# Attention, token mixing and gated net on one core: the token product of the gated net from seven products of quarters, and the work around it in another order

## The reference, cut to what matters

```python
def _moe2_ref(x, w_in, w_spatial, b_spatial, w_out):   # x: 4 x 768 x 384
    h = np.maximum(x @ w_in, 0.0)                       # w_in: 384 x 1024
    u, v = h[..., :512], h[..., 512:]
    v_n = (v - mean(v)) / sqrt(var(v) + 1e-06)          # over the last axis
    v_s = np.einsum('ts,bsd->btd', w_spatial, v_n) + b_spatial[None, :, None]
    return (u * v_s) @ w_out                            # w_out: 512 x 384
```

## Time and profile before

| | us |
|---|---|
| median of 3 runs (lowest, highest) | 599.46 (597.94, 602.70) |
| profiled execution, its own time | 600.73 |
| its span in the profile | 599.0 |
| granted TensorE clock, mean share of full | 0.992 |
| TensorE busy | 582.9 (97%) |
| VectorE busy | 360.4 (60%) |
| ScalarE busy | 283.8 (47%) |

### The profile page before, as it was taken

How to read it: one execution, slowest core, us unless ns; L and a number is a source line. 1 busy time by engine, 2 the same in 40 slices (tenths; PEclk the granted TensorE clock), 3 DMA queues, 4 the chain that set the end, 5 groups by cost and what they waited for, 6 DMA issues and landing times.

```text
span 599.0 us, 11967 instructions
## 1 busy us (share of the span) xinstructions
PE 582.9 (97%) x4248; PEld 557.9 (93%) x4248; DVE 360.4 (60%) x595; ACT 283.8 (47%) x493; POOL 61.4 (10%) x102
## 2 busy tenths in 40 slices
PE   6899999999999999999999999999999999999997
PEld 3788888899999999999999999989999999999996
DVE  6799999677685567447653786555065605570250
ACT  5699999755564244424533635125322523162111
POOL 6366556000000000000000000000000000000000
PEclk9799999999999999999999999999999999999999
DMA  8979999276002130221033540200120010001102
GB/s 192 214 230 244 258 250 337 86 265 250 8 33 63 61 116 13 66 72 48 13 119 127 212 163 2 79 2 1 69 90 1 0 53 26 1 1 40 40 0 82
DMA packets 31115, 58.77 MB, mean 98 GB/s; under 512 B 3680, under 2 KB 23136, under 8 KB 30688
## 3 DMA queue, kind: packets, MB, share of 16 engines
q1 hardware_dynamic: 30816, 57.62, 32.0%
q10 hardware_dynamic: 256, 0.59, 0.4%
HBM read 44.04 MB, written 14.16 MB: 97 GB/s over the span
## 4 chain that ended last, share of the span: by engine, by line
PE 74%; DVE 3%; issue 2%; ACT 1%; DMA 1%; DVEq 0%; ACTq 0%
PE gate_ps L1121 17%; PE theta_bank L1121 11%; PE ringc L1121 11%; PE small_ps L1121 10%; PE mix_ps L1587 8%; PE mix_ps L1592 8%; PE mix_ps L1588 8%; PE small_ps L1551 1%; DVE stats L2119 1%; DVE w_lo L82 1%; DMA x2T<-x 1%; PE mix_ps L1121 1%; DVE vn L2137 0%; DVE x L1785 0%; ACT w_hi L77 0%
## 5 line engine op out<-in xcount | busy, mean ns | idle before, releaser
L1587 PE MATMUL mix_ps<-w_hi,z_hi 128*128 128x384 f32 x288 | 98.6, 342 | 0.0
L1588 PE MATMUL mix_ps<-w_lo,z_hi 128*128 128x384 f32 x288 | 96.6, 336 | 0.0
L1592 PE MATMUL mix_ps<-w_hi,z_lo 128*128 128x384 f32 x288 | 73.5, 337 | 0.0
L1121 PE MATMUL gate_ps<-w_hi 128*128 128x384 f32 x192 | 64.2, 334 | 0.0
L1121 PE MATMUL gate_ps<-w_hi,w_lo 128*128 128x384 f32 x192 | 64.2, 334 | 0.0
L1121 PE MATMUL gate_ps<-w_lo,w_hi 128*128 128x384 f32 x192 | 64.1, 334 | 0.0
L77 ACT ACTIVATE g_hi<-gate 128x384 fp32r<-128x384 f32 x32 | 16.9, 527 | 81.6 <-DVE gate L2169 81.6
L2165 DVE TENSOR_TENSOR gate<-gate_ps,b_all 128x384 f32<-128x384 f32 x32 | 17.8, 557 | 62.5 <-PE gate_ps L1121 62.5
L1587 PEld LDWEIGHTS mix_ps<-w_hi,z_hi 128*128 128x128 f32 x288 | 54.1, 188 | 0.1
L1588 PEld LDWEIGHTS mix_ps<-w_lo,z_hi 128*128 128x128 f32 x288 | 54.2, 188 | 0.0
L1592 PEld LDWEIGHTS mix_ps<-w_hi,z_lo 128*128 128x128 f32 x288 | 51.9, 188 | 0.3 <-DVE z_lo L82 0.3
(11 more groups left out here) (166 smaller groups left out, 1398.9 us busy)
## 6 DMA issues: line engine op xcount, KB each, us to landing
v_raw<-in_vC_dram SPq DMA_DIRECT2D x16, 288.0 KB, 4.9
xT<-y_sb SPq DMA_DIRECT2D x32, 144.0 KB, 4.3
xt<-xT SPq DMA_DIRECT2D x8, 576.0 KB, 4.0
w_raw<-in_wB_dram SPq DMA_DIRECT2D x6, 768.0 KB, 5.7
u<-xT SPq DMA_DIRECT2D x8, 576.0 KB, 5.0
x2T<-x SPq DMA_DIRECT2D x24, 192.0 KB, 1.9
xt<-x2T SPq DMA_DIRECT2D x8, 576.0 KB, 4.7
out_dram<-y SPq DMA_DIRECT2D x24, 192.0 KB, 1.9
```

The costliest lines, as they stand in the source:

```text
L1121: done = pe.matmul(out, a, b, start=(first and n == 0), stop=(last and n == len(terms) - 1))
L1587: pe.matmul(out, z, w_hi[:, weights_of[r]], start=(s == 0 and r == 0), stop=False)
L1588: pe.matmul(out, z, w_lo[:, weights_of[r]], start=False, stop=False)
L1592: last = pe.matmul(out, part(z_lo[i], r * DMODEL + d * 128, 128), w_hi[:, weights_of[r]], start=False, stop=(s == ST - 1 and r == 1))
```

## The change

The product over tokens is cut in halves of tokens in, halves of tokens out and halves of the 512 features, and made of seven products of quarters (the Winograd form of one level of Strassen) where it was eight. `PRODUCTS` names them: each is a values operand (768 columns: 3 token tiles x 256 features) by a weights operand (1152 columns: 3 token tiles x 384). For each product and each 128 features (m) TensorE issues 3 x 3 matmuls of 384 columns into one bank: 7 x 2 x 9 = 126 matmuls for a batch.

- The operands that are sums are made on VectorE: four differences of weights once (`combine`, at the end of the token mixing), four sums of values for each batch (`combine_first_half`, `combine_halves`).
- The values are normalised into one tile, and split only after their sums are there: seven splits of 768 columns on each of ScalarE and VectorE, where there were six of 512. The tile of raw values is the place of their hi parts or lo parts.
- VectorE adds the products up out of PSUM with 22 additions per batch (`add`, bias included), where there were 8, and 8 multiplications by `ut` in place.
- TensorE's order is v(b), output(b-1), u(b), spatial(b), and u sits in the ring's banks after output. ScalarE puts the outputs between the splits of the values, and all of u behind them.
- The next x is loaded into the place of its lo part once u has been made, and split within `gates`; the splits of the gates come after all gates (in the last batch between them).
- The weights for it are loaded in quarters earlier, and four of their eight splits move into the gated net.

```diff
+QUARTER = ST // 2 * HALF
+OPERAND = ST // 2 * FH // 2
+OUT_COLS = FT * DMODEL
+W_AT = {name: n * QUARTER for n, name in enumerate(("t4", "b11", "t1", "b22", "b21", "t3", "t2", "out"))}
+W_ORDER = ("b11", "t2", "b21", "t3", "t1", "t4", "b22", "out")
+V_AT = {name: n * OPERAND for n, name in enumerate(("a11", "s1", "a12", "a22", "s3"))}
+V_TAIL = W_AT["out"] + OUT_COLS
+V_ORDER = ("a11", "s3", "s2", "a12", "s1", "a22", "s4")
+PRODUCTS = (("a11", "b11"), ("s2", "t2"), ("a12", "b21"), ("s3", "t3"), ("s1", "t1"), ("a22", "t4"), ("s4", "b22"))
+SUMS = 22
...
+    def load(self, sp, wC, name):
+        if name == "out":
+            sp.dma_start(self.w_raw[:, self.cols("out")], wC[:, WC_OUT:WC_OUT + OUT_COLS]).then_inc(self.raw_in[name], 16)
+            return
+        s_half, t_half = int(name[1]) - 1, int(name[2]) - 1
+        tokens = wC[:, WC_SP + s_half * ST // 2 * SEQ:WC_SP + (s_half + 1) * ST // 2 * SEQ].rearrange("p (s t) -> p s t", t=SEQ)
+        at = self.cols("t1" if name == "b12" else name)
+        sp.dma_start(self.w_raw[:, at].rearrange("p (s t) -> p s t", t=HALF), tokens[:, :, t_half * HALF:(t_half + 1) * HALF])\
+          .then_inc(self.raw_in[name], 16)
...
+    def difference(self, dve, out, a, b):
+        raw = lambda name: self.w_raw[:, self.cols(name)]
+        dve.tensor_tensor(raw(out), raw(a), raw(b), ALU.subtract).then_inc(self.combined, 1)
+    def combine(self, dve):
+        for name in ("b12", "b22", "b11", "b21"):
+            dve.wait_ge(self.raw_in[name], 16)
+        self.difference(dve, "t3", "b22", "t1")
+        dve.wait_ge(self.combined, 1)
+        self.difference(dve, "t1", "t1", "b11")
+        dve.wait_ge(self.combined, 2)
+        self.difference(dve, "t2", "b22", "t1")
+        dve.wait_ge(self.combined, 3)
+        self.difference(dve, "t4", "b21", "t2")
...
+            def load_spatial(name):
+                def f(b):
+                    if last_batch(b):
+                        if name == "out":
+                            sp.wait_ge(mix_done.h, mix_done.at(b, GROUPS))
+                        else:
+                            sp.wait_ge(mix_used.h, mix_used.at(b, {"b11": 1, "b12": 2, "b22": 3, "b21": 3}[name]))
+                        spatial.load(sp, wC, name)
+                return f
...
+                batches(sp, [(load(0), 0), (load_spatial("out"), 2), (store(0), 2), (load_spatial("b11"), 1), (store(1), 2), (store(2), 2),
+                             (load_spatial("b12"), 1), (load(1), 0), (load_x2, 1), (store(3), 2), (load_spatial("b22"), 1),
+                             (load_spatial("b21"), 1), (store(4), 2), (store(5), 2), (load_residual, 1), (load_w_in, 1)], 2, 1)
...
+            def w_c_combine(b):
+                if last_batch(b):
+                    dve.wait_ge(theta_ps.h, theta_ps.at(b, ST))
+                    dve.wait_ge(mix_used.h, mix_used.at(b, 5))
+                    spatial.combine(dve)
...
-                    (z_down(5), 1), (reduce(0), 0), (multiply(0), 0),
+                    (z_down(5), 1), (w_c_combine, 1), (reduce(0), 0), (multiply(0), 0),
...
+            def value_up(n):
+                name = V_ORDER[n]
+                def f(b):
+                    act.wait_ge(vn_done.h, vn_done.at(b, ST // 2 if name == "a11" else ST))
+                    if name in ("s3", "s1", "s2", "s4"):
+                        act.wait_ge(combined.h, combined.at(b, ("s3", "s1", "s2", "s4").index(name) + 1))
+                    act.wait_ge(vs_ps.h, vs_ps.at(b.back(1), vs_ps.per))
+                    split_hi(act, value_hi(name), value_raw(name)).then_inc(vhi_done.h, 1)
...
+                for o in range(GATES):
+                    act.wait_ge(gated.h, gated.at(b, o + 1))
+                    split_hi(act, g_hi[:, gate_cols(o)], ut[:, gate_cols(o)]).then_inc(ghi_done.h, 1)
+                    if o in (1, 3) and not last_batch(b):
+                        x_hi(b.back(-1), o // 2)
...
-                (v_out(2), 1), (deviation(1), 1), (vn_up(0), 1),
-                (v_out(3), 1), (deviation(2), 1), (vn_up(1), 1),
-                (v_out(4), 1), (deviation(3), 1), (vn_up(2), 1),
-                (v_out(5), 1), (deviation(4), 1), (vn_up(3), 1), (u_out(0), 1), (deviation(5), 1), (vn_up(4), 1),
-                (u_out(1), 1), (vn_up(5), 1), (u_out(2), 1), (u_out(3), 1),
-                (u_out(4), 1), (u_out(5), 1), (u_out(6), 1), (u_out(7), 1),
-                (y_out, 2), (x_hi, 0), (gate_up, 1)], 2)
+                (v_out(2), 1), (deviation(1), 1), (w_up(4), 1),
+                (v_out(3), 1), (deviation(2), 1), (w_up(5), 1),
+                (v_out(4), 1), (deviation(3), 1), (w_up(6), 1),
+                (v_out(5), 1), (deviation(4), 1), (deviation(5), 1),
+                (value_up(0), 1), (y_out(0), 2), (value_up(1), 1), (y_out(1), 2), (value_up(2), 1), (y_out(2), 2),
+                (value_up(3), 1), (y_out(3), 2), (value_up(4), 1), (y_out(4), 2), (value_up(5), 1), (y_out(5), 2), (value_up(6), 1),
+                (u_out(0), 1), (u_out(1), 1), (u_out(2), 1), (u_out(3), 1),
+                (u_out(4), 1), (u_out(5), 1), (u_out(6), 1), (u_out(7), 1), (w_up(7), 1), (gate_up, 1)], 2)
...
-                        pe.wait_ge(v_done.h, v_done.at(b, g + 3))
+                    if g >= 4:
+                        pe.wait_ge(ut_done.h, ut_done.at(b, g - 3))
+                    elif first(b):
+                        pe.wait_ge(v_done.h, v_done.at(b, ST))
                     else:
-                        pe.wait_ge(ut_done.h, ut_done.at(b, g - 3))
...
+            def product(b, n):
+                a, w = PRODUCTS[n]
+                if first(b):
+                    spatial_weights.wait_for(pe, w)
+                pe.wait_ge(vhi_done.h, vhi_done.at(b, V_ORDER.index(a) + 1))
+                pe.wait_ge(vlo_done.h, vlo_done.at(b, V_ORDER.index(a) + 1))
+                for m in range(2):
+                    if n < 2:
+                        pe.wait_ge(summed.h, summed.at(b.back(1), BANK_READ[n + 5][m]))
                     else:
+                        pe.wait_ge(summed.h, summed.at(b, BANK_READ[n - 2][m]))
+                    def values(t, s):
+                        return view(t, v_cols(a).start + s * FH // 2 + m * 128, [[1, 128]])
+                    def weights(t, s):
+                        return part(t, W_AT[w] + s * HALF, HALF)
+                    hi, lo = (v_hi, v_lo) if a in V_AT else (w_hi, w_lo)
+                    three(pe, gate_ps[2 * (n % 2) + m][:, 0:HALF],
+                          [((values(hi, s), values(lo, s)), (weights(w_hi, s), weights(w_lo, s))) for s in range(ST // 2)])\
+                        .then_inc(vs_ps.h, 1)
...
+            batches(pe, [(v_in_ring, 1), (output, 2), (u_in_ring, 1), (spatial, 1)], 2)
...
+            def combine_first_half(b):
+                dve.wait_ge(vn_done.h, vn_done.at(b, ST // 2))
+                dve.tensor_tensor(value_raw("s3"), value_raw("a11"), value_raw("s1"), ALU.subtract).then_inc(combined.h, 1)
+            def combine_halves(b):
+                dve.wait_ge(vn_done.h, vn_done.at(b, ST))
+                dve.wait_ge(combined.h, combined.at(b, 1))
+                dve.tensor_tensor(value_raw("s1"), value_raw("s1"), value_raw("a22"), ALU.add).then_inc(combined.h, 1)
+                dve.wait_ge(combined.h, combined.at(b, 2))
+                dve.tensor_tensor(value_raw("s2"), value_raw("s1"), value_raw("a11"), ALU.subtract).then_inc(combined.h, 1)
+                dve.wait_ge(combined.h, combined.at(b, 3))
+                dve.tensor_tensor(value_raw("s4"), value_raw("a12"), value_raw("s2"), ALU.subtract).then_inc(combined.h, 1)
...
+                for m in range(2):
+                    ps = bank(0, m)
+                    add(left[m], ps, bias(0))
+                    add(right[m], ps, bias(1))
+                for m in range(2):
+                    ps = bank(1, m)
+                    dve.wait_ge(summed.h, summed.at(b, 2 * m + 2))
+                    add(upper[m], ps, left[m][:, :])
+                    add(right[m], ps, right[m][:, :])
+                w_down(5)(b)
+                for m in range(2):
+                    gate(m, left[m], add(left[m], bank(2, m), left[m][:, :]))
+                for m in range(2):
+                    ps = bank(3, m)
+                    dve.wait_ge(gated.h, gated.at(b, m + 1))
+                    dve.wait_ge(summed.h, summed.at(b, 2 * m + 6))
+                    add(left[m], ps, right[m][:, :])
+                    add(upper[m], ps, upper[m][:, :])
+                w_down(6)(b)
+                if last_batch(b):
+                    down(0)
+                    down(1)
+                else:
+                    x_lo(b.back(-1), 0)
+                for m in range(2):
+                    ps = bank(4, m)
+                    dve.wait_ge(summed.h, summed.at(b, 2 * m + 12))
+                    n_sum = add(left[m], ps, left[m][:, :])
+                    add(right[m], ps, right[m][:, :])
+                    gate(2 + m, left[m], n_sum)
```

(20 more changed lines are left out.)

295 lines of the change are left out of this document (147 added, 148 removed).

## The result

| | before | after |
|---|---|---|
| median of 12 runs each, side by side (us) | 599.19 | 596.36 |
| lowest, highest | 597.16, 602.70 | 592.46, 600.09 |
| span of the profiled execution | 599.0 | 595.9 |
| granted clock | 0.992 | 0.989 |

The ratio is 0.9947, with a 95% interval of 0.9922 to 0.9972: about 3 us faster, inside the 1% that the forecast called "within". The medians differ by 2.8 us where the forecast had 3.5; that the time itself is only 0.4 us from the 596.0 predicted says little, since executions of one kernel lie 5.5 (before) and 7.6 us (after) apart.

A forecast was written before the change was run, and what follows sets the result against it. TensorE, busy 582.9 of 599.0 us, bounds the kernel: only fewer matmuls or new pauses matter. -12.5 + 1.75 + 0.35 + 4.85 + 2.3 - 0.85 + 0.6 = -3.5, from the median 599.46 to 596.0 us; range 591.5 to 602.5.

The forecast's parts named there:

- a granted clock of 0.50 behind a pause: Sign of being wrong: TensorE's granted clock at 0.50 behind a pause, where the forecast expected near 0.99.
- Matmuls: Token product: 126 matmuls per batch instead of 144, 72 fewer at 0.1735 us each, -12.5 us, the whole gain.
- The seam: Between mixing and gated net: weight differences delay the first value tiles by 1.75 us and the channel product by 0.35.
- u behind all values: First batch: u's first group waits until all six value tiles are read, +4.85 us.
- u's fifth group: First batch: fifth group waits for the first read into `ut`, behind all seven value splits, +2.3 us (bounds 1.9 and 2.8).
- -0.85: First batch: pauses that u had before vanish, 13.35 us for 72 matmuls that need 12.5.
- Second batch: Three more weight splits on VectorE after the first product make the first output's read 0.3 late, +0.6 us once.
- Later batches: Value tiles are read before output wants their banks, 2.5 us to spare, so no cost.
- Hidden waits: Rival, chance 0.06: banks or engine order leave the pauses out, only the matmuls count, 587.0 us.
- A shorter loop: Rival, chance 0.14: splits and differences fit into gaps, first-batch pauses are 2 and 1.5 us, time 592.3.
- The clock falls in the pause: Rival, chance 0.12: the 4.85 us pause halves TensorE's clock for some 7 us; reaching further, 599 to 603 us.
- Every batch pays: Rival, chance 0.08: VectorE over 2.5 us late at statistics, later batches pay at output and u, 605.6 us.

The follow-up runs named there:

- the additions: Changed kernel with 4, then 9, dependent 384-column VectorE additions at the end of every batch's gates: 601.79 and 611.06 us, one execution each.
- the doubled product: Changed kernel with the 18 matmuls of the first of the seven products issued twice in each batch: 608.06 us, one execution.
- the first experiment: Changed kernel with u taking its old banks in the first batch, so its first group waits only for the third value tile: 601.81 us, one execution.

## Why the prediction was right, point by point

The mechanism was right: the saving of the matmuls, and the places where most of it is lost again. But one of its own signs of being wrong came (a granted clock of 0.50 behind a pause), two terms had the wrong size or the wrong cause, and that the sum came out near is in part luck.

- **Matmuls, -12.5.** Right: 21.89 us for 126 where it was 24.98 for 144, and 12.3 in the stream when 72 are put back.
- **The seam, +1.75 and +0.35.** 1.69 and 0.12 of idle. The differences started at 328.9 (329.1 predicted), took 5.53 to their last one's end (5.4 to its follower's start: 334.35, 334.6 predicted). Taking the cause away gave 2.0.
- **u behind all values, +4.85.** 5.05. The last tile was read at 363.38 (363.1). The walk holds tile by tile: the statistics of tiles 2 to 5 began at 356.18, 359.04, 361.62 and 364.01 where it had 355.9, 358.7, 361.3 and 363.75, each 0.3 later, as the first ones were (352.82 against 352.5).
- **u's fifth group, +2.3.** Right in its end, wrong in its cause: 0.46 of idle. `ut` was there at 372.58 (372.35 predicted), so its time was right; TensorE came to it late, because four groups ran partly at the lower clock. 0.46 + 1.8 = 2.3: the same end by another share, and the table above shows why it could be no less.
- **-0.85, and what is left over.** The first batch as a whole tells: P - M grew by 9.03, where the terms up to there give 8.4. Idle and clock make 1.69 + 0.12 + 5.05 + 0.46 + 1.8 - 0.85 = 8.3; the other 0.7 stands in no idle row but in the starts of the matmuls. An idle row begins when the last matmul ends, 0.16 us after a full stream would have started the next one (358.68 and 0.23 is 358.91, the row of u counts from 359.07): three times 0.16 for the seam, the channel product and u (the fifth group's is in the 1.8). And the matmul behind a pause stands 0.07 to 0.10 further from its follower than in a full stream (336.74 to 337.04 is 0.30, not 0.23): another 0.3 for the three other pauses. A pause costs about 0.25 us more than its idle row says.
- **Second batch, +0.6.** The term that was mis-sized: 1.25 (60.37 from the first product to the second, where the later ones are 59.12 apart). Only 0.23 + 0.18 of it stand in idle rows; about 0.5 is what those two pauses cost beyond their rows, and the rest shorter hold-ups that show in no idle row. From P to the end the change is 216.8 - 228.6 = -11.8, where -12.5 + 0.6 = -11.9 was forecast, but that agreement is luck: behind the last read of the output the trace after is 0.7 shorter, no more than traces of one order differ there.
- **Later batches, nothing.** No pause. The room was 1.5 to 2.0 by the rows and 1.0 to 1.4 by the additions, not 2.5.
- Together: +9.03 - 11.8 = -2.8, and 0.3 from the mixing's earlier end makes the 3.1 between the spans. The forecast was -3.5. Of the 3.1, 1.0 (the end and the mixing) is scatter between two executions; what the two traces show of the change itself is -2.1, give or take the 0.6 by which P - M differs. The medians of 12 executions give -2.8.

The last reads of the output, before (span 599.0) and after (span 595.9):

```profile
594.55 0.49 ACT y L2018
...
592.17 0.49 ACT y L2102
```

**The rivals.** *Hidden waits* is refuted by the idle rows. *A shorter loop* is refuted for the pause (5.05), and tile by tile, since splits and differences cost what the walk had. *The clock falls in the pause* had 0.12 from me, and its first half happened: the granted clock was 0.50 behind the pause, for half as long as in the attention (matmuls stand 0.32 us apart from 364.5 to 367.4, about 3.4 us instead of 7), and its time fell into the next pause, as that rival's text said it would if it began with u. This trace was a mild case: with the doubled product and with 4 and 9 additions, the lower level lasted about 7 us, part of it before u began. Its second half, the reach into the values or the product that would give 599 to 603, did not come. The prediction named the rule of the Trainium skill (TensorE: Matmul & The Clock Gate, HAM oscillation) that idle gaps bring the clock back to half: for the pause of 5.05 us this trace agrees (0.50 from 365 to 367), and I gave too little to it. That the time came out right rests on the cover, and the first experiment shows the price without it: 2.4 us. *Every batch pays* is refuted for the change as it is, and confirmed as a mechanism.

The other rule of the Trainium skill that was weighed (VectorE: DVE Perf Modes, The DRAIN you can't avoid) would have spaced the dependent differences as independent instructions are. Four took 5.53 us, of which the last is 1.35 or so: 1.39 from one to the next, against 1.27 for the splits that do not wait. The row of the dependent pair was the right price, by 0.12 each.

## What to carry to other kernels

Where TensorE is nearly full, cutting matmuls gives exactly their time in the stream, and the reckoning is about the other engines' arrival: here 9.7 of 12.5 us went back by the medians, and by the traces 9.0 in and before the first batch, where no work of an earlier batch fills the waits, and 1.25 in the second. Two pauses on one path are one cost: removing the first alone moved it into the second and lost 2.4 us, removing both gave 6.9, so price a pause by the path that ends it, and test such edits together. And compare traces from a marker near the change: the end of a stage ahead of it lay anywhere within 6 us from run to run here, twice the whole effect, and the end behind it within 1.2 us. Two terms that miss in opposite directions make a sum look right: check each against its own rows.

## What the runs showed of the hardware that was not expected

- The granted clock fell in a pause or with the first work after it. In the trace after it was 1.00 from 359 to 364 with TensorE still, 0.59 and 0.50 from 364 on, 1.00 again at 368. With the doubled product, in the same stretch, it fell while TensorE stood still from 356.3 to 361.6 (the rows behind this list). With 4 additions it was 0.50 from 361, and work began at 362.78; after the pause of 6.75 us it was 0.50 from 373, work began at 374.42, and it was 0.85 from 379 to 381.
- The length of the pause alone did not decide. In one trace, after 2.05 us it stayed near 1.00 for 1.4 us and was then 0.50 from 482 to 485, and after 2.26 us it did not fall at all (1.00 from 543 to 552). After the seam's 1.69 it did not fall either.
- What such a stretch took from the stream varied with it: 1.4 to 2.7 us behind pauses of 4.7 to 5.4, and 2.4 behind the one of 6.75.
- Such a loss can be free or not by what comes next: in the change as it stands the next wait absorbed it, in the first experiment nothing did. The cover is as long as the wait would have been (2.3 us): losses of 1.5 to 2.2 us left the product's start where it was, one of 2.7 moved it by 0.3.
- A pause costs the stream more than its idle row says, by about 0.25 us here: 0.16 between the last matmul's end and where its successor would have started, and 0.07 to 0.10 between the first two matmuls after it.
- A dependent addition of 384 columns costs 0.59 us on VectorE whether it stands between a sum and its gate or in a row of nine (2.95 for five more), so the lateness of an engine can be dosed with it.

The clock in the pause before u, with the doubled product (length, busy us of TensorE, granted clock, DMA share, GB/s):

```profile
358.00:359.00 1.00, 0.00 (x0) 0.83 0.00 0
359.00:360.00 1.00, 0.00 (x0) 0.50 0.00 0
```
